# Channel product in chunks of 512 tokens and one of 256, with its second product interleaved

## What is computed

```python
# x: (batch 4, tokens 576, channels 512)
xt = x.transpose(0, 2, 1)
h = np.maximum(xt @ w_tok1, 0.0) @ w_tok2        # over the tokens, 576 -> 256 -> 576
u = x + h.transpose(0, 2, 1)
h2 = np.maximum(u @ w_ch1, 0.0) @ w_ch2          # over the channels, 512 -> 1536 -> 512
return (u + h2).astype(np.float32)
```

## Time and profile before

| | us |
|---|---|
| median of 3 runs | 1067.08 (1066.78 to 1069.34) |
| the profiled execution, its own time | 1067.29 |
| its span, first to last instruction | 1065.5 |
| TensorE, matmuls busy | 1005.1 (94%) |
| VectorE busy | 595.9 (56%) |
| ScalarE busy | 461.1 (43%) |
| GpSimd busy | 378.1 (35%) |

### The profile page before, as it was taken

How to read it: one execution, slowest core, us unless ns; L and a number is a source line. 1 busy time by engine, 2 the same in 40 slices (tenths; PEclk the granted TensorE clock), 3 DMA queues, 4 the chain that set the end, 5 groups by cost and what they waited for, 6 DMA issues and landing times.

```text
span 1065.5 us, 25232 instructions
## 1 busy us (share of the span) xinstructions
PE 1005.1 (94%) x9616; PEld 870.1 (82%) x9616; DVE 595.9 (56%) x1225; ACT 461.1 (43%) x898; POOL 378.1 (35%) x294
## 2 busy tenths in 40 slices
PE   3899999999999999879999999899999999999998
PEld 2666666666666666659999998888999999999998
DVE  3677777777777777669494948454322212212221
ACT  2677777777777777634151514152211201211210
POOL 3876666666666665531010103286000000000000
PEclk9999999999999999989999999999999999999999
DMA  6344443434344433310000000142000000000000
GB/s 221 91 113 112 111 111 111 111 111 111 111 111 111 111 86 104 119 36 1 1 0 0 0 1 23 30 129 79 1 23 0 22 22 0 22 22 0 22 22 22
DMA packets 34015, 64.80 MB, mean 61 GB/s; under 512 B 4160, under 2 KB 17088, under 8 KB 33984
## 3 DMA queue, kind: packets, MB, share of 16 engines
q1 hardware_dynamic: 33984, 64.37, 21.1%
HBM read 41.81 MB, written 4.72 MB: 44 GB/s over the span
## 4 chain that ended last, share of the span: by engine, by line
PE 66%; issue 21%; DVE 5%; ACT 3%; POOL 2%; DMA 1%; SPq 0%; ACTq 0%; DVEq 0%; POOLq 0%
PE ps L653 12%; PE ps L687 12%; PE ps L688 12%; PE ps L689 12%; PE ps L636 9%; PE ps L595 5%; DVE prob L1052 2%; ACT prob L876 2%; PE ps L624 1%; POOL rstd L557 1%; DVE pT L1067 1%; PE ps L625 1%; PE ps L626 1%; ACT xT L867 1%; DMA stage<-in_moe_w_in 1%
## 5 line engine op out<-in xcount | busy, mean ns | idle before, releaser
L1052 DVE TENSOR_SCALAR_CACHE_REDUCE prob<-ps 128x1152 f32<-128x1152 f32 x144 | 195.5, 1358 | 92.8 <-PE ps L636 72.7
L506 POOL TENSOR_SCALAR prob<-prob,rsum 128x1152 f32<-128x1152 f32 x144 | 176.8, 1228 | 136.5 <-DVE rsum L1061 136.0
L876 ACT ACTIVATE prob<-prob,nmax 128x1152 f32<-128x1152 f32 x144 | 181.4, 1259 | 21.3 <-DVE prob L1052 13.8
L653 PE MATMUL ps<-pT,v_sb 128*64 128x288 f32 x1152 | 170.6, 418 | 14.7 <-ACT xT L867 12.2
L867 ACT ACTIVATE pT<-ps 128x512 f32<-128x512 f32 (+1 forms) x288 | 110.2, 435 | 113.1 <-PE ps L595 112.6
L1015 ACT ACTIVATE f_h<-ps 128x288 fp32r<-128x288 f32 x96 | 39.4, 410 | 245.8 <-PE ps L689 245.8
L636 PE MATMUL ps<-k_over,q_over 64*128 64x288 f32 x768 | 138.2, 313 | 3.5 <-DVE prob L1052 3.5
L636 PEld LDWEIGHTS ps<-k_over,q_over 64*128 64x128 f32 x768 | 108.0, 189 | 23.8 <-DVE prob L1052 22.7
L653 PEld LDWEIGHTS ps<-pT,v_sb 128*64 128x64 f32 x1152 | 71.4, 136 | 56.3 <-issue 18.4
L595 PEld LDWEIGHTS ps<-ident,prob 64*128 64x128 f32 x2592 | 99.7, 140 | 19.7 <-issue 19.7
L687 PE MATMUL ps<-f_h,c_h 128*128 128x288 f32 x384 | 113.7, 296 | 0.0
(11 more groups left out here) (128 smaller groups left out, 2339.4 us busy)
## 6 DMA issues: line engine op xcount, KB each, us to landing
q_raw<-in_q SPq DMA_DIRECT2D x16, 640.0 KB, 4.2
k_raw<-in_k SPq DMA_DIRECT2D x16, 576.0 KB, 4.0
v_sb<-in_v SPq DMA_DIRECT2D x32, 288.0 KB, 2.9
k_over<-kh SPq DMA_DIRECT2D x32, 144.0 KB, 2.5
k_over<-kl SPq DMA_DIRECT2D x32, 144.0 KB, 2.6
out_x<-yT SPq DMA_DIRECT2D x8, 576.0 KB, 3.1
q_over<-qh SPq DMA_DIRECT2D x32, 128.0 KB, 2.2
q_over<-ql SPq DMA_DIRECT2D x32, 128.0 KB, 2.3
```

The costliest lines, as they stand in the source:

```text
L506: g.tensor_scalar(sl, sl, rsum[:, s:s + 1], 0.0, ALU.mult, ALU.add).then_inc(norm_done, 1)
L653: ins = te.matmul(ps[PH * c:PH * c + PH, ACC_BANK, 0:n], v_sb[:, a, j, :], pT[:, a, j, c * n:c * n + n], start=(j == 0), stop=(j == KB - 1))
L876: sc.activation(sl, sl, ACT.Exp, scale=-1.0, bias=nmax[:, s:s + 1], accum_out=esum[:, s:s + 1]).then_inc(exp_done, 1)
L1052: ve.tensor_scalar(prob[:, PROB_BUF[s], :].rearrange("p (c n) -> p c n", c=SCORE_BANKS), ps[:, 0:SCORE_BANKS, 0:CK], -SCALE, BIG, ALU.mult ...
```

## The change

The chunks are laid out anew: one for each batch with its first 512 tokens, and a fifth that gathers the last 64 tokens of all four batches (256 columns, made of four pieces of 64 in `xT`). In each chunk the second product of tile `f` follows the first product of tile `f + 2` (`F_LAG`), and its four output tiles are accumulated side by side in banks 4 to 7. `f_h` and `f_l` keep 4 tiles instead of 12. The sums go back into `xT` in place, `yT` is gone, and the stores read `xT`: four of 1 MB, one for each batch, and at the end four of 128 KB, one for each output tile, with the 64 last tokens of all batches. `u_h`, `u_l`, `f_h` and `f_l` grow to 512 columns. The diff, cut to its core:

```diff
-    out_v = out.rearrange("b (e p) s -> b p e s", p=P)
+    out_v = out.rearrange("b (e p) s -> p (b e) s", p=P)
+    F_N, F_LAG = 4, 2
+    CN = 4 * P
+    LEFT = SQ - CN
...
-        u_h = sb(ctx3b, "u_h", [P, KT_N, HALF], F32R)
...
-        f_h = sb(ctx3b, "f_h", [P, CHT, HALF], F32R)
...
-        yT = sb(ctx3b, "yT", [P, 2, KT_N, HALF])
+        u_h = sb(ctx3b, "u_h", [P, KT_N, CN], F32R)
...
+        f_h = sb(ctx3b, "f_h", [P, F_N, CN], F32R)
...
-        GELU_N, RES_N, F_N, Y_N = 3, 4, 4, 2
+        GELU_N, RES_N, Y_N = 3, 4, 4
...
+        def slab_of(c, e):
+
+            if isinstance(c, int) and c == B:
+                return xT[:, e:NP:KT_N, CN:SQ]
+            return xT[:, c * SPP + e, 0:CN]
...
             with sp.Fori(0, B) as b:
-                for half in range(2):
-                    sp.wait_ge(y_free, at(b, 2 * KT_N, (half + 1) * KT_N + Y_N))
-                    sp.dma_start(out_v[b, :, :, half * HALF:(half + 1) * HALF], yT[:, half, :, :]).then_inc(stored[half], 16)
...
+                sp.wait_ge(y_free, at(b, KT_N, Y_N + KT_N))
+                sp.dma_start(out_v[:, bass.ds(b * KT_N, KT_N), 0:CN], xT[:, bass.ds(b * KT_N, KT_N), 0:CN]).then_inc(stored, 16)
+            for e in range(KT_N):
+                sp.wait_ge(y_free, Y_N + KT_N * B + e + 1)
+                sp.dma_start(out_v[:, e:NP:KT_N, CN:SQ], xT[:, e:NP:KT_N, CN:SQ]).then_inc(stored, 16)
+            sp.wait_ge(stored, 16 * (B + KT_N))
...
+            def first_product(c, f):
+                pe.wait_ge(f_free, at(c, CHT, f + 1))
+                n = B * LEFT if isinstance(c, int) and c == B else CN
+                sl = slice(f * P, (f + 1) * P)
+                for kt in range(KT_N):
+                    if f == 0:
+                        pe.wait_ge(u_split, at(c, KT_N, kt + 1))
+                    ins = three(ps[:, f % F_N, 0:n], c1_h[:, kt, sl], c1_l[:, kt, sl],
+                                u_h[:, kt, 0:n], u_l[:, kt, 0:n], kt == 0, kt == KT_N - 1)
+                ins.then_inc(f_mm, 1)
+
+            def second_product(c, f):
+                pe.wait_ge(f_free, at(c, CHT, F_N + f + 1))
+                n = B * LEFT if isinstance(c, int) and c == B else CN
+                for e in range(KT_N):
+                    if f == 0:
+                        pe.wait_ge(y_free, at(c, KT_N, e + 1))
+                    sl = slice(e * P, (e + 1) * P)
+                    ins = three(ps[:, 4 + e, 0:n], c2_h[:, f, sl], c2_l[:, f, sl],
+                                f_h[:, f % F_N, 0:n], f_l[:, f % F_N, 0:n], f == 0, f == CHT - 1)
+                    if f == CHT - 1:
+                        ins.then_inc(y_mm, 1)
+
             def chunk(c):
...
+                for f in range(CHT + F_LAG):
+                    if f < CHT:
+                        first_product(c, f)
+                    if f >= F_LAG:
+                        second_product(c, f - F_LAG)
+
+            with pe.Fori(0, B) as c:
                 chunk(c)
+            chunk(B)
...
+            def sums(c):
                 for e in range(KT_N):
...
+                    dve.wait_ge(y_mm, at(c, KT_N, e + 1))
+                    ve.tensor_tensor(slab_of(c, e), wide(c, ps[:, 4 + e, :]), slab_of(c, e), ALU.add).then_inc(y_free, 1)
+
+            with dve.Fori(0, B - 1) as c:
+                chunk(c)
+                u_lo_of(c + 1)
+                sums(c)
+            chunk(B - 1)
+            u_lo_of(B)
+            sums(B - 1)
+            chunk(B)
+            sums(B)
```

More of the change, by code:

```diff
@@ L179, in build @@
         ctx3b = ExitStack()
-        u_h = sb(ctx3b, "u_h", [P, KT_N, HALF], F32R)
-        u_l = sb(ctx3b, "u_l", [P, KT_N, HALF], F32R)
-        f_h = sb(ctx3b, "f_h", [P, CHT, HALF], F32R)
-        f_l = sb(ctx3b, "f_l", [P, CHT, HALF], F32R)
-        yT = sb(ctx3b, "yT", [P, 2, KT_N, HALF])
+        u_h = sb(ctx3b, "u_h", [P, KT_N, CN], F32R)
+        u_l = sb(ctx3b, "u_l", [P, KT_N, CN], F32R)
+        f_h = sb(ctx3b, "f_h", [P, F_N, CN], F32R)
+        f_l = sb(ctx3b, "f_l", [P, F_N, CN], F32R)
         ctx3b.close()
@@ L194, in build @@
         small_in = sem("small_in")
-        stored = [sem(f"stored{half}") for half in range(2)]
+        stored = sem("stored")
         ident_zero = sem("ident_zero")
@@ L344, in last_of, with wide @@
             return pT[:, head_of(s), KB - 1, q0:q0 + P].rearrange("p (h q) -> p h q", h=2)
+        def slab_of(c, e):
+            if isinstance(c, int) and c == B:
+                return xT[:, e:NP:KT_N, CN:SQ]
+            return xT[:, c * SPP + e, 0:CN]
+        def wide(c, ap):
+            if isinstance(c, int) and c == B:
+                return ap[:, 0:B * LEFT].rearrange("p (b n) -> p b n", b=B)
+            return ap
         def pT_free(eng, i, s):
@@ L443, in _ @@
             with sp.Fori(0, B) as b:
-                for half in range(2):
-                    sp.wait_ge(y_free, at(b, 2 * KT_N, (half + 1) * KT_N + Y_N))
-                    sp.dma_start(out_v[b, :, :, half * HALF:(half + 1) * HALF], yT[:, half, :, :]).then_inc(stored[half], 16)
-            for half in range(2):
-                sp.wait_ge(stored[half], 16 * ONE + 16 * B)
+                sp.wait_ge(y_free, at(b, KT_N, Y_N + KT_N))
[4 more added lines that the diff above has]
+            sp.wait_ge(stored, 16 * (B + KT_N))
         @block.gpsimd
@@ L836, in _ @@
             pe.wait_ge(w_split, U_END)
-            def chunk(c):
[L839 to L856, removed]
@@ L858, in _ @@
-            with pe.Fori(0, 2 * B) as c:
+            def first_product(c, f):
[8 more added lines that the diff above has]
+                ins.then_inc(f_mm, 1)
@@ L1006, in _, with u_hi_of, chunk @@
             act.wait_ge(u_added, ONE + KT_N)
-            def u_hi_of(b, half):
+            def u_hi_of(c):
                 for e in range(KT_N):
-                    copy(u_h[:, e, :], xT[:, b * SPP + e, half * HALF:(half + 1) * HALF]).then_inc(u_hi, 1)
-            def chunk(b, half, last=False):
+                    copy(wide(c, u_h[:, e, :]), slab_of(c, e)).then_inc(u_hi, 1)
+            def chunk(c):
+                n = B * LEFT if isinstance(c, int) and c == B else CN
                 for f in range(CHT):
[L1014 to L1025, removed]
+                    act.wait_ge(f_mm, at(c, CHT, f + 1))
+                    sc.activation(f_h[:, f % F_N, 0:n], ps[:, f % F_N, 0:n], ACT.Relu).then_inc(f_hi, 1)
+            u_hi_of(0)
+            with act.Fori(0, B - 1) as c:
+                chunk(c)
+                u_hi_of(c + 1)
+            chunk(B - 1)
+            act.wait_ge(u_added, ONE + KT_N * B)
+            u_hi_of(B)
+            chunk(B)
         @block.vector
@@ L1032, in _ @@
             for c, (free, n) in enumerate(((gelu_done, GELU_N), (res_done, RES_N), (f_free, F_N), (y_free, Y_N),
[L1033 removed]
+                                            (h1_lo, ONE), (u_added, ONE))):
                 ve.memset(scrap[:, c:c + 1], 0.0).then_inc(free, n)
@@ L1233, in tokens_lo, with u_lo_of @@
                                      ALU.subtract).then_inc(xn_lo, 1)
-            def u_lo_of(b, half):
+            def u_lo_of(c):
                 for e in range(KT_N):
-                    dve.wait_ge(u_hi, at(b, 2 * KT_N, half * KT_N + e + 1))
-                    ve.tensor_tensor(u_l[:, e, :], xT[:, b * SPP + e, half * HALF:(half + 1) * HALF],
-                                     u_h[:, e, :].bitcast(F32), ALU.subtract).then_inc(u_split, 1)
+                    dve.wait_ge(u_hi, at(c, KT_N, e + 1))
+                    ve.tensor_tensor(wide(c, u_l[:, e, :]), slab_of(c, e), wide(c, u_h[:, e, :]).bitcast(F32), ALU.subtract)\
+                        .then_inc(u_split, 1)
             def token_mix(b, last):
@@ L1249, in token_mix @@
                 else:
-                    u_lo_of(0, 0)
+                    u_lo_of(0)
                 for f in range(KT_N):
@@ L1264, in _, with chunk @@
             dve.wait_ge(u_added, ONE + KT_N * B)
-            def chunk(b, half, last=False):
+            def chunk(c):
+                n = B * LEFT if isinstance(c, int) and c == B else CN
                 for f in range(CHT):
-                    dve.wait_ge(f_hi, at(b, 2 * CHT, half * CHT + f + 1))
-                    ve.scalar_tensor_tensor(out=f_l[:, f, :], in0=ps[:, f % F_N, 0:HALF], scalar=0.0,
-                                            in1=f_h[:, f, :].bitcast(F32), op0=ALU.max, op1=ALU.subtract)\
+                    dve.wait_ge(f_hi, at(c, CHT, f + 1))
+                    ve.scalar_tensor_tensor(out=f_l[:, f % F_N, 0:n], in0=ps[:, f % F_N, 0:n], scalar=0.0,
+                                            in1=f_h[:, f % F_N, 0:n].bitcast(F32), op0=ALU.max, op1=ALU.subtract)\
                         .then_inc(f_free, 1)
-                if not last:
-                    u_lo_of(*((b, 1) if half == 0 else (b + 1, 0)))
+            def sums(c):
                 for e in range(KT_N):
[L1275 to L1286, removed]
+                    dve.wait_ge(y_mm, at(c, KT_N, e + 1))
```

(10 more changed lines are left out.)

## The result

The changed kernel took 1053.14 us in the median (1053.07 to 1053.23, 4 runs) beside 1066.93 us for the kernel before (1065.16 to 1069.34, 4 runs): a ratio of 0.9869, 95% interval 0.9850 to 0.9889. Two later comparisons of the same two kernels, with more runs of the kernel before, gave 0.9887 (0.9872 to 0.9902, 1055.09 against 1067.24 us) and 0.9894 (0.9877 to 0.9911, 1055.36 against 1067.35 us), 12 us. So there are two things to explain: 12 us in place of 10.5, and why the first comparison showed 14.

What follows compares the result with a forecast made beforehand. TensorE's issue of matmuls was taken to bound the last stage. -11.5 us for fewer matmuls, 0 for three other terms and +1.0 for the end made -10.5, taking the median 1067.08 to 1056.6 us; range 1054.3 to 1061.0.

Steps and rivals of the forecast that it cites:

- The price of a small packet: Last four stores, 256-byte packets: between 11 ns, in proportion to bytes, and 51 ns each, as for 1152 bytes.
- what lies ahead of the stage: Everything before the channel stage: no term in the sum; the stage should start near 754, as in the profile before.
- Fewer, wider matmuls: Channel stage: 1440 matmuls instead of 2304, each with 13.3 ns independent of width, so 295.7 us against 307.2, -11.5 us.
- More changes of bank: Channel stage: 172 more changes of bank for TensorE's matmuls, taken to cost 0, at most 0.3 us.
- The waits of the interleaved product: Channel stage, second product: `f_l` needs 1.7 us and other blocks cover 10.9 to 2.9 us, so waits cost 0.
- the last batch of the product over the tokens: Just before the channel stage: wider `u_l` subtractions delay the first addition, with 0.2 us left; cost 0, perhaps +0.3 us.
- The end: Last matmul to last store landed: four stores of 256-byte packets, between -1.3 and +4.0 us, taken as +1.0 us.
- A: Rival, the ends cost more: 256-column matmuls at 0.1333 (1060.4 us) or last stores at 51 ns a packet (1059.6); chance 0.12.
- B: Rival, channel stage: wide matmuls slow down beside VectorE, 0.2325 us each at 512 columns, 1063.3 us; chance 0.07.
- C: Rival, channel stage: the 13.3 ns follow the columns, so wider matmuls save nothing, 1068.1 us; chance 0.03.
- D: Rival, second product: TensorE waits for a fresh `f_l` and its clock falls, 1134 us; chance 0.04.
- E: Rival, better than forecast: 256 columns at 0.109 us, or small packets at 11 ns with it, about 1053 us; chance 0.04.

## Why the prediction was wrong, point by point

Two steps failed. The price of a small packet was set too high, which is 1.55 us of the sum; and what lies ahead of the stage was put at nothing, which is 2.05 us in the first comparison.

- **Fewer, wider matmuls: right to the tenth.** Forecast 261.1 and 34.6 us, -11.5; measured 261.13 and 34.43, -11.50. The line through 288 and 512 columns also gave the width that no row had, 256. It does not hold for all widths: at 384, 448 and 480 columns the part above 0.4167 ns a column is 15.2, 16.0 and 16.5 ns instead of 13.3.
- **More changes of bank: right**, no cost to be seen.
- **The waits of the interleaved product, and the last batch of the product over the tokens: right.** TensorE has no wait in either, and the first addition there ends in time. One tile of lag in place of two would have done.
- **The end: wrong, the term of the sum that was mis-sized.** +1.0 us was taken and -0.55 measured. The step read the landing of 512 tiny packets, 3.0 us, as a sign that packets hardly get cheaper with their bytes. Here they do: 18 ns for 256 bytes and 27 for 512, beside 51 for 1152. Those three lie near a line of 9 ns and 0.036 ns a byte. The tiny ones were also queued behind another load, so their landing was no measure of a packet. With -0.55 the sum is 1055.0 us, against 1055.09 and 1055.36 in the two later comparisons, which lie inside the range. The Trainium skill ("DMA: Bandwidth & Descriptors", section "Specifications") has such transfers below line rate, and the trace agrees: 0.52 MB in 2.38 us is 220 GB/s, against 0.59 MB in 1.69 us, 350 GB/s, for the 1152-byte ones; those of 512 bytes, which that section has at line rate, come to 1.05 MB in 3.62 us, 290 GB/s, and there the measurement decides. The 256-byte packets were still cheaper than what was assumed.
- **What lies ahead of the stage: wrong, put at nothing without a word.** This is what took the first result out of the range, since -12.05 alone is inside it. The sum was made against one execution that had a low-clock stretch near the end of the gated block, and took that as fixed. In the first comparison's profile the stage starts 2.05 us earlier, 1.52 of them with that stretch gone. The runs of the kernel before already lay between 1066.78 and 1069.34 us, up to 2.3 us from their median; a range widened by that much on either side would have reached 1052.0.
- **Rivals.** A and B did not happen: 256 columns ran at 0.1200, 512 at 0.2267. C is refuted by the same numbers. D was tried: with no cover the waits come and cost 95.7 us, but the clock stays at 1.00 through 60 waits of 1.3 us in the mean, so the second half of D is refuted for waits of this length. The Trainium skill ("TensorE: Matmul & The Clock Gate", section "A second HAM failure mode: psum-queue depth-cycling") tells of a clock lost to short idle times between groups of matmuls; no run here shows that in the stage, neither with the banks changing and no wait (granted clock 1.00) nor with these waits. Of E, the cheap packets came half true (-0.55 us of at most -1.3), the faster 256 columns did not. Its terms of -3.1 and -2.3 us make 1053.5 and 1051.2, where it has "about 1053" for both; that the first result, 1053.14, lies near that number is chance.

## What to carry to other kernels

Where one engine issues back to back, divide the work by the number of its instructions: the fixed part of each, read as the difference of paces at two widths, is what wider instructions save (13.3 ns x 864 here), and the wanted width is worth a run, since 448 and 480 columns did worse than 512 and 256 together. Interleaving a dependent product frees buffers (4 tiles in place of 12), which leaves room for wider ones; whether the wide chunk would have fitted without it was not tried. The order alone shortened the stage by 1 us, and a lag of one tile was enough. Before pricing a few us, look how far apart the runs of the kernel before lie, and put that in the range.

## What was not expected of the hardware

- The pace of a 128 x 128 fp32r matmul with its own weight load, at the full clock: 256 columns 0.1200 us, 288 0.1333, 384 0.1752, 448 0.2027, 480 0.2165, 512 0.2267. The fixed part is 13.3 ns at 256, 288 and 512 and 15.2 to 16.5 ns at the three others. Why was not found; at 448 the buffers had the same row length as at 512, so it is not that. At the lower clock 288 columns took 0.240, which is 288 / 1.2 GHz with nothing on top.
- With the products interleaved, 288 columns ran at 0.1329 us instead of 0.1333, 1.0 us over the stage; the cause stays open.
- Waits of 1.3 us in the mean after every 24 matmuls, all through the stage, left the granted clock at 1.00. In the gated block it fell after TensorE had been busy 2.42 of 4 us, and not in every execution, with the same instructions: that is worth 1.5 us of this kernel's time. The run with a lag of one tile was busy just as long there and kept the full clock, so this alone doesn't tell when it falls:

```profile
672.00:676.00 4.00, 2.42 (x19) 2.19 (x17) 2.64 (x4) 0.68 (x1) 0.00 (x0) 1.00 0.12 47
676.00:680.00 4.00, 3.83 (x29) 3.59 (x29) 1.13 (x2) 0.00 (x0) 0.00 (x0) 1.00 0.02 4
```
